# Attention, an MLP and a top-1 mixture of experts on one core: the experts after the first in units of 32 tokens on four column groups of TensorE

## What is computed

```python
# q, k, v: (4, 8, 576, 64); block-causal attention, block 64
x = softmax(mask(q @ k.T / 8)) @ v            # -> x: (2304, 512)
h = x @ w_in; g = max(0.01 * h, h)            # d_ff 2048
x = g @ w_out                                 # (2304, 512)
do = x @ w_skip > 0                           # tokens that are computed at all
e_idx = argmax(x @ w_gate, axis=1)            # 8 experts, top 1
gate_w = softmax(x @ w_gate)[e_idx]
for e in range(8):                            # w1[e]: (512, 1024), w2[e]: (1024, 512)
    y[mask_e] = gate_w * (relu(x[mask_e] @ w1[e]) @ w2[e])
out = x.copy(); out[do] = x[do] + y
```

## Time and profile before

| | us |
|---|---|
| median of the three timed runs | 755.23 |
| span of the profiled execution, first to last instruction | 751.5 |
| what the timed median has beyond that span | 3.7 |
| start of the first tile on PE | 613.1 |
| end of PE's last matmul | 746.1 |
| PE, ACT, DVE, POOL busy | 737.1, 295.6, 358.6, 144.0 |

### The profile page before, as it was taken

How to read it: one execution, slowest core, us unless ns; L and a number is a source line. 1 busy time by engine, 2 the same in 40 slices (tenths; PEclk the granted TensorE clock), 3 DMA queues, 4 the chain that set the end, 5 groups by cost and what they waited for, 6 DMA issues and landing times.

```text
span 751.5 us, 12647 instructions
## 1 busy us (share of the span) xinstructions
PE 737.1 (98%) x4358; PEld 594.2 (79%) x4359; DVE 358.6 (48%) x761; ACT 295.6 (39%) x674; POOL 144.0 (19%) x190
## 2 busy tenths in 40 slices
PE   7999999999999999999999999999999999999997
PEld 4556877778877887898888787878887878999984
DVE  6776554465546442013355456465655252352641
ACT  5566655555445543234432223222221131332450
POOL 3136554333222221100020000000000032222121
PEclk9999999999999999999999999999999999999999
DMA  4335766645555532475766566565652117777773
GB/s 128 99 125 166 228 194 197 181 128 152 145 161 143 145 88 73 104 209 169 196 179 188 165 201 171 172 187 157 183 164 91 57 44 237 245 214 245 222 229 96
DMA packets 97537, 121.60 MB, mean 162 GB/s; under 512 B 13842, under 2 KB 60706, under 8 KB 97480
## 3 DMA queue, kind: packets, MB, share of 16 engines
q1 hardware_dynamic: 94664, 116.50, 53.0%
q0 software_dynamic: 1920, 3.77, 1.7%
q10 hardware_dynamic: 896, 0.59, 0.2%
HBM read 89.09 MB, written 31.31 MB: 160 GB/s over the span
## 4 chain that ended last, share of the span: by engine, by line
PE 94%; issue 2%; DVE 1%; ACT 1%; DMA 1%; POOL 0%; SPq 0%; DVEq 0%; POOLq 0%; ACTq 0%
PE ps_h L1728 9%; PE ps_x L1815 9%; PE ps_x L1817 9%; PE ps_x L1816 9%; PE ps_hid L1987 9%; PE ps_h L1730 9%; PE ps_h L1729 8%; PE ps_o L1711 6%; PE ps_t L1685 5%; PE ps_y L1998 2%; PE ps_y L2000 2%; PE ps_y L1999 2%; PE ps_s L1636 2%; PE ps_s L1672 2%; PE ps_s L1673 2%
## 5 line engine op out<-in xcount | busy, mean ns | idle before, releaser
L1728 PE MATMUL ps_h<-xh,win_h 128*128 128x512 f32 (+1 forms) x320 | 122.7, 383 | 1.3 <-ACT act L1084 1.1
L1730 PE MATMUL ps_h<-xh,win_l 128*128 128x512 f32 (+1 forms) x320 | 118.4, 370 | 0.0
L1729 PE MATMUL ps_h<-xl,win_h 128*128 128x512 f32 (+1 forms) x320 | 118.0, 369 | 0.0
L1815 PE MATMUL ps_x<-wout_h,g_hi 128*128 128x512 f32 x288 | 114.0, 396 | 0.0
L1817 PE MATMUL ps_x<-wout_h,g_lo 128*128 128x512 f32 x288 | 112.3, 390 | 0.0
L1816 PE MATMUL ps_x<-wout_l,g_hi 128*128 128x512 f32 x288 | 112.1, 389 | 0.0
L1070 ACT ACTIVATE prob<-ps_s,neg_max 128x128 f32<-128x128 f32 (+3 forms) x144 | 78.9, 550 | 54.8 <-DVE neg_max L1291 38.2
L1291 DVE TENSOR_REDUCE neg_max<-ps_s 128x1 f32<-128x128 f32 (+3 forms) x144 | 71.0, 509 | 58.4 <-PE ps_s L1673 35.6
L1084 ACT ACTIVATE act<-ps_h 128x512 f32<-128x512 f32 (+1 forms) x80 | 44.3, 555 | 124.1 <-PE ps_h L1730 119.3
L1331 DVE TENSOR_TENSOR g_lo<-g_raw,g_hi 128x512 fp32r<-128x512 f32 x72 | 49.4, 687 | 58.3 <-ACT g_hi L1094 58.1
L1728 PEld LDWEIGHTS ps_h<-xh,win_h 128*128 128x128 f32 x320 | 60.4, 189 | 11.6 <-issue 1.4
(11 more groups left out here) (205 smaller groups left out, 1095.4 us busy)
## 6 DMA issues: line engine op xcount, KB each, us to landing
g_raw<-hidden SPq DMA_DIRECT2D x72, 256.0 KB, 3.8
hidden<-act SPq DMA_DIRECT2D x64, 256.0 KB, 2.4
w_sb<-in_w SPq DMA_DIRECT2D x32, 512.0 KB, 5.0
w_two<-in_w SPq DMA_DIRECT2D x32, 512.0 KB, 5.0
k_raw<-in_k_t SPq DMA_DIRECT2D x40, 144.0 KB, 3.1
x2rows<-x SPq DMA_DIRECT2D x18, 256.0 KB, 2.4
out<-x SPq DMA_DIRECT2D x18, 256.0 KB, 2.6
w_stage<-in_w_in SPq DMA_DIRECT2D x16, 256.0 KB, 3.0
```

Source lines behind the costliest of these rows:

```text
L1728: e.matmul(dst, win_h[:, f, kc, :], xh[m][:, kc, :], start=kc == 0, stop=False)
L1729: e.matmul(dst, win_h[:, f, kc, :], xl[m][:, kc, :], start=False, stop=False)
L1730: last = e.matmul(dst, win_l[:, f, kc, :], xh[m][:, kc, :], start=False, stop=kc == KC - 1)
L1815: e.matmul(dst, hi, wout_h[:, f, :], start=f == 0, stop=False)
```

## The change

Expert 0 keeps its loop of 128-token tiles. Experts 1 to 7 go in units of 32 tokens, floor(n/32)+1 for each, one PE loop per expert, the total made even. `x2` is stored a third time, as quarter rows: 4 rows of 132 numbers per token (128 values and the gate weight), so that one gather of 128 quarter rows gives a unit already laid out as (quarter, token) on the partitions. One transpose turns it. In the first product the tokens are stationary (32 columns) and `w1` moves: each of the four column groups makes 256 hidden columns for the 32 tokens. One ReLU, two transposes, two copies; then the second product, each group 128 output columns.

```diff
@@ SP
+            def store_quarters(t):
+                e.dma_start(quarters[P * t:P * (t + 1), :, 0:P], x2[...] as "p c d").then_inc(s_wd[m % 2], 16)
+            def store_lane_weights(m):
+                for c in range(KC):
+                    e.dma_start(quarters[m * BLK:(m + 1) * BLK, c, P:Q_W]..., x2[m % 2][:, :, DM:ROW_W])...
             def load_expert(x, n):
-                if done > 0:
-                    e.wait_ge(loaded, 16 * done)
...
+            for x in (2, 3):
+                for n in range(LOADS):
+                    load_expert(x, n)
+            e.wait_ge(m_y, tiles + 1)           # then expert 4
+            for x in range(5, E):
+                past = first_unit(e, x - 3)
+                e.wait_ge(q_y, past)
...
@@ POOL
-            for x in range(E):
-                e.tensor_copy(order[:, bass.ds(starts[x], SLOTS)], idx[:, x * SLOTS:(x + 1) * SLOTS])...
+            gather_unit(0, 0)
+            gather_unit(1, 1)
             rows_free(0)
             gather(1)
...
+            with e.Fori(0, pairs) as pair:
+                for odd in range(2):
+                    u = 2 * pair + odd
+                    e.wait_ge(q_next, u + 2)
+                    gather_unit(u + 3, 1 - odd)
+                    scatter_unit(u, odd)
@@ ACT
+            with e.Fori(0, pairs) as pair:
+                for odd in range(2):
+                    u = 2 * pair + odd
+                    e.wait_ge(q_held, u + 1)
+                    e.wait_ge(q_out, u + 1)
+                    e.copy(kept_q[:, :], row_q_now[:, :]).then_inc(q_kept, 1)
+                    e.wait_ge(q_rt, u + 1)
+                    e.wait_ge(q_kept, u + 1)
+                    hold_unit(u + 1)
+                    relu_unit(u)                # one activation, 128x256
+                    e.wait_ge(q_ht, 2 * u + 2)
+                    e.copy(hid_tq[:, 1, :], ps_ht[1][:, 0:P]).then_inc(q_rest, 1)
+                    e.wait_ge(q_held, u + 2)
+                    next_unit(pair + 1, odd)    # waits for the gather
@@ DVE, after base_f
+            ...                                 # tiles_0, steps_to, ends_i, reached, weighed,
+            ...                                 # pairs_f, column, pairs_i: nine short instructions
+            for lane in range(4):
+                for quarter in range(4):
+                    e.tensor_scalar(to[:, :, quarter], idx[own, SLOTS:E * SLOTS], float(KC), float(lane), ...)
+            tiles = first_tiles(e)
+            pairs = unit_pairs(e)
+            e.tensor_copy(columns[0:1, :], ps_cnt[0:1, P:P + COLS])...
+            unit_gather(0, 0)                   # value load and index copy
+            unit_gather(1, 1)
             move_rows_t(0)
...
+            def unit(pair, odd):
+                e.wait_ge(q_gather[1 - odd], (pair + odd + 1) * 16)
+                unit_gather(u + 3, 1 - odd)
+                e.wait_ge(q_ht, 2 * u + 1)
+                e.tensor_copy(hid_tq[:, 0, :], ps_ht[0][:, 0:P]).then_inc(q_first, 1)
+                move_unit_t(u + 1)
+            def unit_out(pair, odd):
+                e.tensor_copy(scatter_q[odd][:, :], listed_at(u)).then_inc(q_sidx, 1)
+                e.wait_ge(q_y, u + 1)
+                e.wait_ge(q_kept, u + 1)
+                e.scalar_tensor_tensor(out=y_q[odd][:, :], in0=ps_y[:, 0:P], ...).then_inc(q_out, 1)
@@ PE, in place of the loops of experts 1 to 7
+            for x in range(1, E):
+                e.wait_ge(s_w1[x], 16 * KC)
+                for loaded in s_w2[x]:
+                    e.wait_ge(loaded, 16 * (LOADS - KC))
+                with e.Fori(firsts[x - 2] if x > 1 else 0, firsts[x - 1]) as u:
+                    e.wait_ge(q_rows, u + 1)
+                    for k in range(KC):
+                        for c, own in enumerate(lanes):
+                            f = 2 * c * P
+                            last = e.matmul(ps_hid[0][own, 0:2 * P], rows_tq[:, lanes[k]], w1_of(x)[:, k, f:f + 2 * P],
+                                            start=k == 0, stop=k == KC - 1)
+                    last.then_inc(q_hid, 1)
+                    transpose_unit(u + 1)
+                    e.wait_ge(q_relu, u + 1)
+                    e.transpose(ps_ht[0][:, 0:P], hid_q[:, 0, :], ident[:, :]).then_inc(q_ht, 1)
+                    e.transpose(ps_ht[1][:, 0:P], hid_q[:, 1, :], ident[:, :]).then_inc(q_ht, 1)
+                    e.wait_ge(q_first, u + 1)
+                    e.wait_ge(q_out, u + 1)
+                    for half in range(2):
+                        if half:
+                            e.wait_ge(q_rest, u + 1)
+                        for k in range(4):
+                            for c, own in enumerate(lanes):
+                                last = e.matmul(ps_y[own, 0:P], hid_tq[:, half, lanes[k]],
+                                                w2_of(x)[:, 2 * k + half, P * c:P * c + P], ...)
+                    last.then_inc(q_y, 1)
```

More of the change, by code:

```diff
@@ L376, in build @@
         base_f = sb("base_f", [P, E + 1])
[L378 to L392, removed]
-        below = sb("below", [P, E + 1, E])
[L394 to L397, removed]
+        part_i = sb("part_i", [P, 1], I32)
@@ L398, in build @@
+        sb("gap", [P, GAP])
+        sb("next_two", [P, 2 * EXPERT_W])
         w2_hi = sb("w2_hi", [P, EC, DM], F32R)
-        hid_early = sb("hid_early", [P, EC, P])
         hid_hi = sb("hid_hi", [P, EC, P], F32R)
         hid_lo = sb("hid_lo", [P, EC, P], F32R)
-        y_out = sb("y_out", [P, DM])
-        order = sb("order", [P, MAX_TILES + 2 * SLOTS], I32)
+        rows = sb("rows", [P, ROW_W])
+        idx = sb("idx", [P, E * SLOTS], I32)
+        listed = sb("listed", [P, LISTED], I32)
@@ L425, in build @@
         ps_rt = ps("ps_rt", BANK)
+        ps_ht = [ps(f"ps_ht{i}", BANK) for i in range(2)]
         s_const = sem("s_const")
@@ L1008, in gather @@
             def gather(g):
[L1009 removed]
+                e.tensor_copy(gather_at[:, :], idx[:, bass.ds(g, 1)]).then_inc(m_gidx, 1)
                 e.wait_ge(m_gidx, g)
@@ L1026, in _ @@
             scatter()
-            with e.Fori(0, total_tiles) as g:
+            with e.Fori(0, tiles) as g:
                 rows_free(g + 1)
@@ L1965, in _ @@
             early_hidden(27, EC * KC)
-            starts = []
+            firsts = []
             for f in range(EC):
+                if f == 6:
+                    e.wait_ge(s_column, 1)
+                    e.matmul(ps_cnt[0:1, P:P + COLS], column[:, :], ident[:, 0:COLS],
+                             start=True, stop=True).then_inc(s_colrow, 1)
                 if f == EC - 1:
@@ L2004, in _ @@
-            loaded_to(e, SHARED, W_LOADS - 1)
-            e.wait_ge(s_second, 2)
-            with e.Fori(starts[SHARED], starts[E]) as g:
-                second = e.value_load(second_i[0:1, bass.ds(g, 1)], min_val=0, max_val=1)
+                    tiles = first_tiles(e)
+                if 3 <= f <= 5:
+                    firsts.append(first_unit(e, 2 * f - 4))
+                    firsts.append(first_unit(e, 2 * f - 3))
+                if f == 6:
+                    firsts.append(2 * unit_pairs(e))
```

436 lines of the change are left out of this document (269 added, 167 removed).

## The result

| | before | changed |
|---|---|---|
| median of the runs, us | 755.12 (754.36 to 756.22, 4 runs) | 759.57 (758.73 to 760.56, 4 runs) |
| ratio to before | | 1.0059, 95% interval [1.0044, 1.0073] |
| span of the profiled run, us | 751.5 | 756.9 (its time 758.92) |

Slower by 0.6%, where the sum gave 754.1 us, 0.15% faster. The page's busy times, to set beside the earlier trace rows: TensorE (PE) has 11 us less to do, and still the span is 5 us longer.

A forecast was written before the change was run, and what follows sets the result against it. PE, busy 98% of the span, was taken as the bound. Units start at 654.4 us, 18 units add 90.9, the end brings the span to 750.4, and 3.7 for median over span gives 754.1 us; range 748.5 to 768.

The forecast's parts named there:

- What lies beside it: ACT, DVE and POOL work within a unit: all fit, POOL tightest at 3.9 of 5.05 us; gathers issued early.
- the waits between loads of one place go: SP's weight loads lose their pacing waits during the units; claimed only to help, no size given.
- rival 1: A gap in PE's own program in each unit, 0.45 us, unit 5.5: 762.2 us, slower; 33%.
- the list of signs: Profile signs of error: PE idle "issue" in each unit, POOL or gathers releasing ACT, first unit waiting for loads.
- The unit: Chain of PE's steps and waits for one unit: 5.05 us, 1.5 of it waits; 18 units 90.9 us.
- Rival 3: The column groups don't keep pace in a long series: unit 11.9 us, kernel 878 us; 3%.
- Ahead of the tiles: New DVE work before `rows_t`: first tile at 614.3 us, 1.2 later than before; bounds 613.1 and 615.4.
- Time less span: Timed median taken as 3.7 us above the profiled span, added at the end to reach 754.1 us.
- Projection: Extra stores during the projection stage cost 0, bounds 0 and 4 us, as the DMA engines had free time.
- The loads: SP's 48 weight loads in series: expert 7's end at about 738 us, its unit starts at 740, so hidden.
- The end: Behind the units, from 745.3 us: y, last scatter, and 2.6 us after POOL's last instruction; span 750.4.
- Rival 4: The clock falls because PE idles 1.5 of 5 us in a unit: 1.2 GHz, 821 us; 2%.

The follow-up runs named there:

- e1_early: Changed kernel with the third unit's row numbers, copies and gather moved ahead of expert 0's tile loop; 752.85 us, ratio 0.9973.
- e7_late_loads: Changed kernel with expert 4's loads held until the second unit's second product is done; 760.90 us, ratio 1.0077.
- e2_paced: Changed kernel with the loads of experts 2 to 7 again waiting for the load before the last; 756.83 us, ratio 1.0031.
- e3_quarters: Kernel before, with only the third store of x2 (quarter rows) and the 24 small gate weight stores added; 754.43 us, ratio 0.9997.
- e9_one_wait: Changed kernel with the early third gather, and PE's wait inside the second product moved ahead of it; 760.01 us, ratio 1.0078.
- e8_again: The changed kernel itself, unedited, timed again on another chip; 765.70 us, ratio 1.0134.

## Why the prediction was wrong

**The step that failed** is in "What lies beside it": "Gathers are issued more than a unit ahead. So all three fit." It fails for the third unit, and the wait for its rows, with the clock that fell behind it, cost 5.2 us that the sum has at nothing. The first two units' gathers go out before expert 0's tiles. The third unit's stands in GpSimd's program behind the last tile's scatter, and its row numbers in VectorE's behind the last tile's `y_out`. Its buffer had long been free: ScalarE's first `next_q` ran at 651.5. The gather went out 2.66 us after the first unit had begun, and PE wanted its rows turned at 663.6, 4.1 us later; they took 7.2. The prediction took a steady unit as good for the first ones. Linked to it is "the waits between loads of one place go, which can only help". They can hurt: 16 loads in two bursts fill the DMA engines (share 1.02 to 1.04) just when a gather that PE needs is under way. e1_early removes the first cause and with it the whole stall; e7_late_loads removes the second and leaves about 1 us at most; e2_paced restores the waits and gets back a little under half.

The measured time lies within the stated range, 748.5 to 768, and even in the band of rival 1. That is luck: rival 1's gap isn't in this profile, and no rival has a gather that comes late. Only the list of signs does ("if POOL or the gathers release ACT"), without a price.

Term by term, against the profiled run of the changed kernel:

| | predicted, us | measured, us |
|---|---|---|
| start of the first unit | 654.4 | 656.8 |
| of it, `idx` later than before | 0 | 2.6 |
| of it, the first tile's own delay | 1.2 | 1.1 |
| 18 units | 90.9 | 88.2 |
| the stall | 0 | 5.2 |
| end of the units to end of the span | 5.1 | 6.8 |
| span | 750.4 | 756.9 |
| time less span | 3.7 | 2.0 |

- **The unit**: right, 4.90 for 5.05. Both products came as costed (1.84 and 1.77 us from start to what follows, for 1.75 and 1.78), and the two waits of 0.24 and 0.27 us are the ones named. Rival 3 is out: 64 pairs in the four groups take 1.75 us, about 27 ns each. The Trainium skill's figure of about 81 ns a pair at 128 columns (TensorE: Matmul & The Clock Gate, Back-to-back issue gap) doesn't carry over to four groups side by side; this kernel measures a third of it.
- **Ahead of the tiles**: right in sum, 16 `listed` being dearer (4.84 for 4.0) and the rest cheaper. Of the other 2.6 us in the table most are not the change's: 1.2 of them stand already at 283 us, in attention, and e3_quarters, which has no units, has `idx` 1.6 us later than before at an unchanged time. The upper bound of 615.4 was passed by them, too: the first tile came at 616.9.
- **Time less span**: 3.7 was no property of the kernel. It set the median of three runs beside the span of one. Every later run of "before" has its own span on record, and its time stands 1.7 to 1.8 us above it; so the profiled execution, with 751.5, was some 1.9 us faster than the median, and starting from it made the start of the units too early by about as much as 3.7 is too large. The two cancel in the sum.
- **Projection**: right, by e3_quarters and by the window at 540 us, where PE is busy 20.00 of 20.00.
- **The loads**: hidden, as forecast, but not in one series as in the earlier trace rows. They come in bursts of eight or sixteen as places in the arena (the buffer that holds the weights) come free, and PE waits for none.
- **The end**: 1.7 us more than forecast, since the last scatter lasts 4.3 us behind POOL's last instruction, not 2.6.
- **Rival 4, the clock**: it didn't fall in a regular unit, as forecast. It fell in the stall, from about 667.9 to 671.3 us.
- **Rival 1, a gap in PE's program**: absent in the profile of the first measurement, and there on two of the chips, if the pauses with "issue" are that gap, which isn't shown: 5.15 to 5.2 us instead of 4.90 in nearly every unit, 18 times 0.25 to 0.3. With it the changed kernel stands at 1.0125 to 1.0134; and the version without the stall is 1.004 instead of 0.9973 to 0.9981.

With the failed step mended, the sum came out near: e1_early is 1.9 us below before, where -1.1 was forecast. Part of that is luck, as the units are 2.7 us cheaper than forecast and the end 1.7 dearer.

**What stays open** is the cause of the longer units on two of the chips. Shown is that the same program has them in one group of runs and not in another, for all kernels with units of a group alike, that PE pauses with nothing released, that full DMA engines aren't needed for it, and that the long pauses come without the wait in the middle of the product, too. As no chip was used in two groups, the chip can't be told from the time at which a group ran. That PE gets its instructions more slowly there would fit, but half and twice the pairs, made to test it, ran twice on chips without the effect. In e9_one_wait the time moved within the unit and did not get less.

## What to carry to other kernels

When a loop is put behind another and is fed through buffers that rotate, check the first trips one by one: the last transfer that is issued before the first loop, and the next one, which comes late however well the steady state fits. Here its buffer was free in good time, and only its place in the program held it. A wait that paces large loads is also a reservation for small transfers; before taking it away, list the transfers that fall into the burst and what stands in order behind their reader. And where a chain of short steps saves little, measure on several chips: here a gain of 0.2 to 0.3% on three is a loss of 0.4% on a fourth.

## What the runs showed of the hardware

- A gather of 128 quarter rows landed 3.5 us after its issue at the median (2.2 to 7.6 in the changed kernel). At the place of the stall it took 7.2 us under 16 loads of 512 KB at 406 to 418 GB/s (7.5 in e8_again), 4.9 with the loads paced (e2_paced), and 4.2 without them (e7_late_loads).
- The granted clock went to 0.50 behind an idle time of 4.1 us on PE, and in e2_paced behind one of 1.7 us; the second product of 1.96 us then took 3.10 and 3.35. So the shorter wait cost no less by the clock than the longer one. Waits of 0.24 and 0.27 us in each unit left it at 1.00.
- Four column groups of 32 made 64 pairs of weight load and matmul of 128 columns in 1.75 us, 27 ns a pair, against 112 ns over the full width.
- Two of six groups of runs had the unit 5 to 6% longer at a granted clock of 1.00. The kernel before, with 128-token tiles alone, took 754.4 to 755.2 us in all of them, so one kernel can differ from chip to chip, or from time to time, where another doesn't.
